# Routed expert stage of a fused attention, MLP and expert kernel: first expert's weight load split around its gather, rows turned earlier, search steps placed later, last products reordered

## What is computed

```python
# 1: decayed linear attention, state by state over 768 steps
for t in range(S):
    cur = np.einsum('bhd,bhe->bhde', u[None] * kt, vt)
    y[:, :, t] = np.einsum('bhd,bhde->bhe', rt, state + cur)
    state = w[None, :, :, None] * state + np.einsum('bhd,bhe->bhde', kt, vt)
# 2: MLP with a learned leak, 3072 x 384 -> 2048 -> 384
h = x @ w_in
x = (np.maximum(h, 0.0) + alpha * np.minimum(h, 0.0)) @ w_out
# 3: 8 experts, each takes 384 tokens, greedily by the largest logits first
order = np.argsort(-(x @ w_gate).flatten())
for idx in order:
    tok, e = (int(idx) // E, int(idx) % E)
    if assigned[tok] >= 0 or counts[e] >= cap:
        continue
    assigned[tok] = e
    counts[e] += 1
for e in range(E):
    mask = assigned == e
    out[mask] = np.maximum(x[mask] @ w1[e], 0.0) @ w2[e]
```

## Time and profile before

| | us |
|---|---|
| median of 3 runs | 814.81 (814.66 to 815.09) |
| the profiled execution, its time | 814.79 |
| its span | 813.0 |
| TensorE busy | 771.2 (95%) |
| VectorE busy | 501.1 (62%) |
| GpSimd busy | 473.2 (58%) |
| ScalarE busy | 220.5 (27%) |

### The profile page before, as it was taken

The page is one execution under the profiler, slowest core; times in us unless marked ns, Lnnn a source line. Parts: engine busy times, 40 slices in busy tenths (PEclk is TensorE's granted clock), DMA queues, the critical chain, the costliest instruction groups (busy, mean ns, idle before and its releaser), DMA issues.

```text
span 813.0 us, 15976 instructions
## 1 busy us (share of the span) xinstructions
PE 771.2 (95%) x6325; PEld 650.4 (80%) x6325; DVE 501.1 (62%) x1039; ACT 220.5 (27%) x452; POOL 473.2 (58%) x468
## 2 busy tenths in 40 slices
PE   6899999999999999999999999838899999999996
PEld 4678788888888888888888888625788988989996
DVE  7987666556655666556554433477787777776121
ACT  1333322111211121112112111104244344344351
POOL 6899975555555555555553333109376775775871
PEclk8999999999999999999999999859999999999998
DMA  8865422222222222221000000023524505508401
GB/s 228 228 192 156 144 60 69 69 69 69 70 69 69 69 69 65 68 65 40 11 10 11 10 11 10 29 87 118 185 61 155 213 27 190 188 27 286 141 21 39
DMA packets 46649, 75.17 MB, mean 92 GB/s; under 512 B 6256, under 2 KB 31984, under 8 KB 46576
## 3 DMA queue, kind: packets, MB, share of 16 engines
q1 hardware_dynamic: 37920, 56.27, 21.8%
q10 hardware_dynamic: 5584, 8.46, 3.6%
q0 software_dynamic: 3072, 9.44, 3.2%
HBM read 64.71 MB, written 9.44 MB: 91 GB/s over the span
## 4 chain that ended last, share of the span: by engine, by line
PE 77%; DVE 11%; POOL 6%; issue 2%; DMA 2%; ACT 2%; SPq 0%; POOLq 0%; DVEq 0%; ACTq 0%
PE bank L1253 22%; PE bank L1255 21%; PE bank L1254 21%; PE bank L1304 3%; PE bank L1270 3%; POOL gl L474 2%; PE bank L1287 2%; PE bank L1363 2%; DVE grid L1148 2%; PE bank L1446 2%; DMA raw<-w 1%; POOL wout_l L418 1%; DVE grid L1146 1%; POOL win_l L418 1%; DVE both L819 1%
## 5 line engine op out<-in xcount | busy, mean ns | idle before, releaser
L474 POOL TENSOR_TENSOR gl<-g,gh 128x512 fp32r<-128x512 f32 x96 | 128.2, 1335 | 204.6 <-ACT gh L640 204.6
L962 DVE TENSOR_SCALAR q<-bank,alpha_sb 128x512 f32<-128x512 f32 x96 | 71.9, 749 | 147.8 <-PE bank L1255 147.5
L640 ACT CAST gh<-g 128x512 fp32r<-128x512 f32 x96 | 59.6, 621 | 339.2 <-PE bank L1255 303.3
L1253 PE MATMUL bank<-gh,wout_h 128*128 128x512 f32 x288 | 118.6, 412 | 1.2 <-DVE vs L846 0.5
L1253 PE MATMUL bank<-xTh,win_h 128*128 128x512 f32 x288 | 113.1, 393 | 0.3 <-DVE xTl L855 0.3
L1255 PE MATMUL bank<-gh,wout_l 128*128 128x512 f32 x288 | 112.8, 392 | 0.0
L1254 PE MATMUL bank<-gl,wout_h 128*128 128x512 f32 x288 | 112.4, 390 | 0.0
L1255 PE MATMUL bank<-xTh,win_l 128*128 128x512 f32 x288 | 112.2, 389 | 0.0
L1254 PE MATMUL bank<-xTl,win_h 128*128 128x512 f32 x288 | 112.1, 389 | 0.0
L572 POOL TENSOR_TENSOR w1l<-raw,w1h 128x384 fp32r<-128x384 f32 x64 | 64.9, 1014 | 32.9 <-ACT w2h L704 31.6
L1253 PE MATMUL bank<-xeh,w1h 128*128 128x384 f32 x192 | 69.8, 363 | 0.9 <-DVE xel L1079 0.9
(11 more groups left out here) (191 smaller groups left out, 1472.1 us busy)
## 6 DMA issues: line engine op xcount, KB each, us to landing
raw<-w SPq DMA_DIRECT2D x32, 768.0 KB
rt<-rT SPq DMA_DIRECT2D x48, 96.0 KB, 2.7
vs<-v SPq DMA_DIRECT2D x48, 96.0 KB, 2.9
vn<-v SPq DMA_DIRECT2D x24, 192.0 KB, 2.9
x2rows<-x2n SPq DMA_DIRECT2D x24, 192.0 KB, 1.9
kt<-kT SPq DMA_DIRECT2D x44, 96.0 KB, 2.5
kn<-kN SPq DMA_DIRECT2D x20, 192.0 KB, 2.5
rn<-rN SPq DMA_DIRECT2D x20, 192.0 KB, 2.6
```

The lines of the kernel that those rows point to most:

```text
L474: nc.gpsimd.tensor_tensor(gl[:, f % 2], g[:, f % 2], gh[:, f % 2].bitcast(F32), ALU.subtract).then_inc(gl_ready, 1)
L640: nc.scalar.copy(gh[:, f % 2], g[:, f % 2]).then_inc(gh_ready, 1)
L962: nc.vector.tensor_scalar(q[:, f % 2], h, 0.0, alpha_sb[:, f:f + 1], ALU.min, ALU.mult).then_inc(q_ready, 1)
L1253: nc.tensor.matmul(o, a_h, b_h, start=first, stop=False)
```

## The change

SyncE loads the first halves of w1 and w2 of the first expert, then waits for the three gathers, then loads the second halves. The last of the 24 stores to `x2rows` moves from SyncE to GpSimd as an indirect DMA, and the first `is_ar` moves from VectorE to GpSimd. In chunk 0 GpSimd does `decay2(1, 2)` and `padded_keys(1, 3)` ahead of two weight pieces. The tables for the first three bodies are new, and the lists of ScalarE and VectorE follow them. For the last expert all hidden blocks come first, and the nine last parts are reordered by row block; its last hidden block has buffers of its own (`last_gh`, `last_gl`).

```diff
-                    store(c, b)
+                    if (c, b) != (NCH - 1, B - 1):
+                        store(c, b)
...
                 for c in range(2):
+                    if p == 0 and c == 1:
+                        for a in range(NA):
+                            sp.wait_ge(gathered[a], 16)
                     sp.dma_start(raw1[:, par, :, c * hf:(c + 1) * hf],
...
                     if other is not None:
                         other(f)
+                    if i == 0 and f == 9:
+                        decay2(1, 2)
+                        padded_keys(1, 3)
                     if late:
...
+            pool.wait_ge(rows_known, 1)
+            pool.wait_ge(x2n_ready, NT + OUT_PRE)
+            nc.gpsimd.indirect_dma_start(x2rows, bass.IndirectOffsetOnAxis(ap=last_rows_at[:, 0:1], axis=0), x2n[:, 1], None).then_inc(last_stored, 16)
...
+            pool.wait_ge(last_stored, 16)
+            pool.wait_ge(rows_marked, 1)
+            nc.gpsimd.tensor_tensor(is_ar[:], is_a[:], rowid[:].unsqueeze(2).to_broadcast([P, NT, NS]), ALU.mult).then_inc(rows_numbered, 1)
...
-            hi(0, range(5))
-            rows_hi(0, 0)
-            hi(0, range(5, 6))
-            rows_hi(0, 1)
-            rows_hi(0, 2)
-            hi(0, range(6, NF2))
+            hi(0, range(NF2 // 2))
+            for a in range(NA):
+                rows_hi(0, a)
...
                 relu_hi(p, 0)
+                if p == 0:
+                    hi(0, range(4, 5))
                 if p >= 1:
                     rows_out(p - 1)
-                    hi(p, range(7, 8))
+                    hi(p, range(4, 6) if p == 1 else range(7, 8))
                 relu_hi(p, 1)
+                if p == 0:
+                    hi(0, range(5, NF2))
+                if p == 1:
+                    hi(1, range(6, NF2))
...
-                if p == 1 and m == 3:
-                    for a in range(NA):
-                        rows_lo(0, a)
+                if p == 1 and m == 2:
+                    rows_lo(0, 0)
+                    rows_lo(0, 1)
...
-                counts_at = (2, 5, 10, 20, 25, 29) if new == 0 else (3, 7, 12, 17, 21, 25) if new == 1 else (2, 7, 11, 16, 21, 25)
+                counts_at = ((2, 5, 18, 23, 27, 31), (7, 11, 15, 19, 23, 27), (3, 7, 12, 17, 21, 25))[new] if new < 3 else (2, 7, 11, 16, 21, 25)
...
-                turns_at = (7, 8, 9) if new == 0 else (7, 9, 11) if new == 1 else (5, 7, 10)
-                busy_at = {0: 9, 2: 2, 4: 4, 5: 2, 6: 1, 7: 1, 8: 1, 10: 4} if new == 0 else {}
+                turns_at = ((4, 4, 5), (9, 11, 13), (7, 9, 11))[new] if new < 3 else (5, 7, 10)
+                busy_at = {0: 9, 2: 2, 4: 4, 5: 2, 6: 1, 7: 1} if new == 0 else {}
...
-            for s in range(done[0], 6 * NF2 * E - 3):
+            for s in range(done[0], 6 * NF2 * E - 9):
                 stream(s)
-            for f, a in ((NF2 - 2, 0), (NF2 - 2, 1), (NF2 - 1, 0), (NF2 - 2, 2), (NF2 - 1, 1), (NF2 - 1, 2)):
+            for k in range(KD):
+                expert_hidden(E - 1, NF2 - 1, k)
+            for f, a in ((5, 0), (6, 0), (5, 1), (7, 0), (6, 1), (7, 1), (5, 2), (6, 2), (7, 2)):
                 expert_back(E - 1, f, a)
```

More of the change, by code:

```diff
@@ L165, in build @@
         xel = sb("xel", [P, 2, KD, CAP], F32R)
+        last_gh = sb("last_gh", [P, CAP], F32R)
+        last_gl = sb("last_gl", [P, CAP], F32R)
         consts_loaded, u_loaded, wcol_set = sem("consts_loaded"), sem("u_loaded"), sem("wcol_set")
@@ L274, in build, with hidden_h, hidden_l @@
         KNOWN = NT - B
+        def hidden_h(p, f):
+            return last_gh[:] if (p, f) == (E - 1, NF2 - 1) else gh[:, f % 2, 0:CAP]
+        def hidden_l(p, f):
+            return last_gl[:] if (p, f) == (E - 1, NF2 - 1) else gl[:, f % 2, 0:CAP]
         def turned_rows(p, a):
@@ L487, in chunk @@
                             prepare(1, b + 1)
-                        elif not (i == 0 and f < 9):
+                        elif not (i == 0 and f < 10):
                             if f % 4 == 1:
@@ L707, in relu_hi @@
                 act.wait_ge(h2_done, NF2 * p + f + 1)
-                wait(act, ffn_out_done, NF2 * p + f - 1)
-                nc.scalar.activation(gh[:, f % 2, 0:CAP], banks[3 + f % 2][:, 0:CAP], ACT.Relu).then_inc(g2h_ready, 1)
+                if (p, f) != (E - 1, NF2 - 1):
+                    wait(act, ffn_out_done, NF2 * p + f - 1)
+                nc.scalar.activation(hidden_h(p, f), banks[3 + f % 2][:, 0:CAP], ACT.Relu).then_inc(g2h_ready, 1)
             def rows_hi(p, a):
@@ L724, in rows_out @@
                     nc.scalar.copy(yg[:, a], banks[a][:, 0:DM]).then_inc(yg_ready, 1)
-            hi(0, range(5))
-            rows_hi(0, 0)
-            hi(0, range(5, 6))
-            rows_hi(0, 1)
-            rows_hi(0, 2)
-            hi(0, range(6, NF2))
-            for p in range(E):
-                if p >= 1:
+            hi(0, range(NF2 // 2))
+            for a in range(NA):
+                rows_hi(0, a)
+            for p in range(E):
+                if p == 1:
+                    hi(1, range(0, 1))
+                    relu_hi(0, 5)
+                    hi(1, range(1, 2))
+                    relu_hi(0, 6)
+                    rows_hi(1, 0)
+                    rows_hi(1, 1)
+                    relu_hi(0, 7)
+                    rows_hi(1, 2)
+                    hi(1, range(2, 4))
+                if p >= 2:
                     hi(p, range(0, 1))
@@ L1071, in relu_lo @@
                 dve.wait_ge(g2h_ready, NF2 * p + f + 1)
-                V.scalar_tensor_tensor(out=gl[:, f % 2, 0:CAP], in0=banks[3 + f % 2][:, 0:CAP], scalar=0.0, in1=gh[:, f % 2, 0:CAP].bitcast(F32),
+                V.scalar_tensor_tensor(out=hidden_l(p, f), in0=banks[3 + f % 2][:, 0:CAP], scalar=0.0, in1=hidden_h(p, f).bitcast(F32),
                                        op0=ALU.max, op1=ALU.subtract).then_inc(g2l_ready, 1)
@@ L1111, in while_counting @@
             def while_counting(p, m):
-                if p == 1 and m == 3:
-                    for a in range(NA):
-                        rows_lo(0, a)
+                if p == 1 and m == 2:
+                    rows_lo(0, 0)
+                    rows_lo(0, 1)
                 if p == 1 and m == 4:
                     relu_lo(0, 0)
-                if p >= 2 and m == 1:
+                if p == 2 and m == 2:
+                    relu_lo(0, 6)
+                    rows_lo(1, 0)
+                if p == 2 and m == 3:
+                    rows_lo(1, 2)
+                    relu_lo(0, 7)
+                if p == 2 and m == 6:
+                    relu_lo(1, 1)
+                if p >= 3 and m == 1:
                     relu_lo(p - 2, 5)
-                if p >= 2 and m == 2:
+                if p >= 3 and m == 2:
                     rows_lo(p - 1, 0)
-                if p >= 2 and m == 3:
+                if p >= 3 and m == 3:
                     relu_lo(p - 2, 6)
                     rows_lo(p - 1, 2)
-                if p >= 2 and m == 4:
+                if p >= 3 and m == 4:
                     relu_lo(p - 2, 7)
-                if p >= 2 and m >= 5:
+                if p >= 3 and m >= 5:
                     relu_lo(p - 1, m - 5)
             def while_placing(p, m):
+                if p == 1 and m == 2:
+                    rows_lo(0, 2)
+                if p == 2 and m == 4:
+                    relu_lo(1, 0)
                 if p >= 2 and m == 2:
@@ L1217, in route @@
                     start_key(slice(0, NT))
+                if p == 1:
+                    relu_lo(0, 5)
             front(slice(KNOWN, NT))
@@ L1500, in inverse @@
             def inverse(p, half):
-                pe.wait_ge(inverse_ready, 3 * p + 2 + half)
+                pe.wait_ge(inverse_ready, 3 * p + 1 + half)
+                if p == 0 and half == 0:
+                    pe.wait_ge(rows_numbered, 1)
                 for j in range(half * NT // 2, (half + 1) * NT // 2):
@@ L1533, in expert_back @@
                 rows = slice(a * P, (a + 1) * P)
-                mm = product3(banks[a][:, 0:DM], gh[:, f % 2, rows], gl[:, f % 2, rows], w2h[:, f], w2l[:, f], f == 0, f == NF2 - 1)
+                mm = product3(banks[a][:, 0:DM], hidden_h(p, f)[:, rows], hidden_l(p, f)[:, rows], w2h[:, f], w2l[:, f], f == 0, f == NF2 - 1)
                 if p == E - 1 and f == NF2 - 1:
```

31 lines of the change are left out of this document (20 added, 11 removed).

## The result

The changed kernel takes 808.71 us (median of 4 runs, 808.28 to 809.85), the kernel before 814.73 beside it (813.45 to 815.09): ratio 0.9929, 95% interval 0.9917 to 0.9942. The forecast was 807.3, range 805.6 to 811.0. So 6.0 us are gone where 7.5 were forecast. The profiled execution of the changed kernel is the slowest of the four, 809.85, with a span of 808.1; the kernel before had 813.0.

What follows compares the result with a forecast made beforehand. The prediction took TensorE to bound the kernel (77% of the chain), only matmuls costing time once the experts run. Its sum was 814.8 - 0.95 - 3.1 - 2.2 - 1.3 = 807.3 us, range 805.6 to 811.0.

Steps and rivals of the forecast that it cites:

- Chunk 0: In chunk 0, GpSimd makes kpad earlier, so TensorE's wait for it goes: -0.95 us.
- The end at 0: Other limit for chunk 0: the wait comes back two blocks later as a wait for a weight piece, gain 0.
- The start of the stream: The first expert's stream of products starts at 556.4 instead of 559.49: -3.1 us.
- I count nothing for that: At the stream's start, no gain counted for the first gather's longer issue (1.18 against 0.95) and late start.
- The other end: At the stream's start, the gather lands with its old 5.0, everything behind it 1.8 later: only -1.3 us.
- the slower case: Rival: second halves landing later than 563.0 hold up ScalarE, TensorE and the search; gains used up at 570.5; chance 0.03.
- The rivals of the late gathers and the clock: Two rivals: gathers land as late as before, 809.2, chance 0.09; clock grant falls back at waits, 808.6, chance 0.05.
- The waits in the first two bodies: TensorE's waits for the search in the first two bodies fall from 6.2 to 4.0: -2.2 us.
- Of the third body's 31.6 us I change nothing: The third body was taken to keep its length of 31.6 us.
- the first rival: The search takes the waits back, so the gain of 2.2 in the first two bodies is 0: 809.5, chance 0.18.
- The end: At the kernel's end, 0.28 of idle time goes and the third scatter is issued at 806.55, not 807.86: -1.3 us.
- if these counts are further apart: Sign of a wrong prediction: first counts of the third and fourth body more than 31.6 us apart.

Runs made afterwards that it cites:

- chunk0_back: Changed kernel with GpSimd's old order in chunk 0, two weight pieces ahead of decayed and kpad: 809.99 us, ratio 0.9944 to the kernel before.
- store_back: Changed kernel with the last store back on SyncE and the first is_ar back on VectorE: 808.84 us, ratio 0.9929 to the kernel before.
- no_load_wait: Changed kernel without SyncE's wait for the three gathers before the second halves of the first expert's weights: 812.69 us, ratio 0.9975 to the kernel before.
- third_steady: Changed kernel with the slots of the fourth and later bodies used in the third body too: 807.42 us, ratio 0.9915 to the kernel before.
- steps_later: third_steady with the third to sixth search step one slot later from the third body on: 806.53 us, ratio 0.9902 to the kernel before.
- tail_back: Changed kernel with the old order of the last products, the last hidden block's own buffers kept: 808.98 us, ratio 0.9939 to the kernel before.

## Why the prediction was right, and where it was not

**Chunk 0** (-0.95): -1.1 in the trace of before against four of the changed kernel's kind, -1.2 by chunk0_back. Right. The end at 0, that the wait comes back, did not happen.

**The start of the stream** (-3.1): B went from 16.0 to 12.6, -3.4. Right in size, and partly by luck. The step "I count nothing for that" (the first indirect DMA's extra) was wrong: store_back gives 0.7 for it together with the `is_ar`, for which 0.2 was counted, and without the two the term would be -2.7. The other end, "everything behind it is 1.8 later", was wrong more: I took the old landing of 5.0 as the worst, though that gather had been issued when the loads were two thirds through, and the one before it had taken 5.8 in the same trace. Issued earlier, it meets more of them: 6.4, and with TensorE's clock 4.0 in all. The wait on SyncE holds that off, so the forecast stood. Second halves at 559.5, before the 563.0 of the slower case; the clock was 0.97 from 550 to 560. The rivals of the late gathers and the clock did not come in the changed kernel, but no_load_wait shows both, the second behind the waits that the first makes: 3.0 and 1.0.

**The waits in the first two bodies** (-2.2): this is the step that failed, in one sentence of it. The walk up to there was right: part 83 at 54.9 and 55.0 after the start in the two traces, 54.8 forecast, 57.0 before. "Of the third body's 31.6 us I change nothing" was not: from part 83 to the first count of the fourth body it takes 33.1, 1.8 more. Its table had changed too: it got the slots 3, 7, 12, 17 that the second body had had, and with them their waits, 0.52, 0.37, 0.23, 0.37. I had walked two bodies and stopped where the third began, at the point where the waits were handed on. The net of the term is -0.2 (88.1 from the stream's start to the first count of the fourth body, 88.3 before), near the 0 of the first rival: the measured 808.7 lies nearer to its 809.5 than to 807.3. But its reason, that the search itself holds TensorE, is only half of it: third_steady and steps_later take 2.1 us out by slots alone, so there was room in the search.

**The end** (-1.3): from the first count of the fourth body to the last instruction 165.2 became 164.0, -1.2; tail_back gives 1.4. Right.

**The sum**: -1.1 - 3.4 - 0.2 - 1.2 = -5.9, and the medians say -6.0 and -6.4. The forecast had one term two microseconds too large, two a little too small and one right within 0.1; because of the first the sum promised 1.1 to 1.5 too much. Of what would make it wrong the prediction named "if these counts are further apart", and that is what happened: 32.6 instead of 31.6 from the third body's first count to the fourth's.

## What to carry to other kernels

In a pipeline whose order is a table, walk the change until the schedule is again the same as before, entry by entry, and not only to where the edit seems to end: a wait that leaves one round may stand in the next. A small transfer that starts a long chain may land much later when it is issued beside bulk loads (6.5 us instead of 3.0 here), and its worst landing is not the one that an old trace shows, but the one at the moment of its new issue. Hold the bulk back, and take what waits for the bulk out of the small one's way on every engine: one without the other left the start of the stream at 16.7 or 20.2 us, where it was 16.0 before and 12.6 with both.

## What was not expected of the hardware

- A gather of 128 rows of 1.5 KB lands 3.0 to 3.6 us after its issue when it is issued in the last 3 us of two loads of 768 KB or behind them, 5.0 and 5.8 towards the end of four loads, and 6.4 to 6.5 in the middle of them.
- GpSimd's first indirect DMA of the program takes 1.17 to 1.20 us instead of 0.95 to 1.01. Where it is a gather it starts 1.26 and 1.31 behind the row numbers, a later one 0.61. It need not be the one that matters.
- `decayed` on GpSimd took 0.83 in its old place and 1.28 in its new one, and the split of hidden values 1.30 or 1.75 from block to block. In the second trace of the changed kernel the 1.29 of `decayed` begins at 86.75, while VectorE's `both_odd`, a product of two SBUF tiles, runs from 86.29 to 87.36; and the 1.75 begins at 91.16, while VectorE's `kt` runs from 90.40. Where `both_odd` begins second, at 127.73, `decayed` (from 127.69) keeps its 0.83 and `both_odd` takes 1.34 instead of 0.91. So in these places the one that begins second is the longer one; no run tried it alone.
- TensorE, with waits of 1.68 and 0.73 between 551.3 and 554.3, was granted half its clock from 555 to 558 (no_load_wait).
